# An attention and expert kernel on one core: code of k ahead of the products with v, additions and roundings of VectorE in two-input form, first heads in another order

## The chip, the cores and the metric

The kernel runs on one core of a Trainium2 chip. The metric is the device time of one execution in microseconds (us), the median of the runs shown. Five engines work side by side, each through its own queue in order, and wait for one another by semaphores: TensorE (PE; PEld are its weight loads), VectorE (DVE), ScalarE (ACT), GpSimd (POOL) and SyncE (SP, which only issues transfers here).

## What is computed

Attention over 16 heads (2 batches of 8), 768 rows of 64 each, in which a row of q sees only those rows of k whose six sign bits under a random projection are the same; then a layer of 8 experts with one expert per token; then a dense layer with ELU. The change touches the attention alone.

```python
q_bits = (np.einsum('bhsd,dk->bhsk', q, proj) > 0)      # 6 bits a row; k_bits likewise
mask = q_bucket[:, :, :, None] == k_bucket[:, :, None, :]
scores = np.where(mask, scale * q @ k.T, -1e9)
scores = scores - scores.max(-1)
attn = np.exp(scores); attn = attn / (attn.sum(-1) + 1e-09)
x = attn @ v          # then the experts, then moe2
```

## The kernel before

**Tiling.** A head has six score tiles of 128 rows (J = 6, HALF = 384 columns are one bank). Tile m is computed by `scores(m)` into pair_s or pair_t (L1202, eight matmul records, as fp32r high and low parts q_a, q_b, k_a, k_b), VectorE takes its negated maximum (`row_max`, L850), ScalarE the exponential with its row sum (`exp_rows`, L643), TensorE turns it (`turn_exps`, L1213, six transposes in two halves of three), ScalarE copies the first half out (`copy_t0`, L652) and VectorE the second (`copy_t1`, L873), and TensorE multiplies by v (`times_v`, L1228, 12 matmuls for half a head) and by the last weights (`last`, L1250).

**Preparing a head.** `project(g)` (L1172) makes the bits, `sign(g)` (L857, VectorE) makes them 0 or 1, `code(g, 0)` for q and `code(g, 1)` for k (L1184, TensorE) turn them into a code in bank_a (k's code of heads 0 and 1: bank_b). The code is read out by `mask_odd` on ScalarE (L628 for q, L630 for k) and `mask_even` on VectorE (L865). `high(g, c)` on VectorE (L843, L841) rounds q (c = 0) and k (c = 1) to fp32r; GpSimd copies and subtracts the roundings (`place_q`: L504, L506; `place_k`: L513, L515), scales k (L528), works on finished rows (`rows_of`, L487 to L495) and subtracts weight chunks (`w_lo`, L476).

**Denominators.** `inverse(u)` (VectorE) adds 1e-9 to the row sums den (L879, 128x6 values) and takes the reciprocal (L880).

**Order.** After a start written out by hand, a loop over n = 6 to 53 has three parts per head g = n // 3, each with two score tiles of head g - 1. The same loop stands on every engine, so that each queue's order is fixed. In part 1 of head g TensorE had: scores twice, `turn_exps(m_e)`, `times_v`, `turn_exps(m_e + 1)`, `code(g, 1)`. VectorE had in part 1: `copy_t1`, `mask_even(g, 0)`, `row_max` twice, `copy_t1`, `high(g + 1, 1)`, `mask_even(g, 1)`, `inverse(g - 2)`, and in part 2 first `copy_t1`, then `row_max`. `code(g, 1)` waits for both readers of `code(g, 0)`, since both codes lie in bank_a. `turn_exps(m)` waits for the first half before its first transpose, and for `copy_t1(m - 1)` before its fourth.

**Start.** `WARM_UP` is the number of matmuls on zeros (L1270) ahead of `project(0)` and ahead of `scores(0)`. `scores(0)` waits for all masks of head 0 and for the parts of q and k.

Of the kernel before, what the change touches and what calls it, by code (L numbers as in the profile page):

```python
# [22 lines left out]
ALU = mybir.AluOpType  # L23
# [10 lines left out]
EPS = 1e-9  # L34
# [5 lines left out]
HEADS = B * H  # L40
# [27 lines left out]
GROUPS = 3 * (HEADS + 2)  # L68
GROUP_S, GROUP_E = 3, 4
COPIES = 4  # L70
WARM_UP = (7, 10)
BIT_K = 32
BT = 3
NB = BT * P
# [56 lines left out]
def program(nc, q, k, v, proj, w_gate, w_ogate, w1, w2, w_in, w_out, const, out):  # L131
    with ExitStack() as ctx:
# [31 lines left out]
        with ExitStack() as att:  # L164
# [10 lines left out]
            raw = sb("raw", [P, 2, S])  # L175
# [94 lines left out]
        def turned_tile(m, part):  # L270
            a = (m // JH % 4) * HALF + m % JH * P
            return exps_t[:, part, a:a + P]
# [14 lines left out]
        s_hi, s_qa, s_ka = sem("s_hi"), sem("s_qa"), sem("s_ka")  # L287
# [185 lines left out]
        def _(pool):  # L473
# [41 lines left out]
                pool.tensor_tensor(k_b[top, g % 3, :], raw[low, g % 2, :], k_b[low, g % 3, :].bitcast(F32),  # L515
                                   ALU.subtract).then_inc(s_cp, 1)

            pool.wait_ge(s_hi, 1)
            pool.tensor_tensor(q_b[low, 0, :], raw[top, 0, :], q_b[top, 0, :].bitcast(F32), ALU.subtract).then_inc(s_cp, 1)
            pool.wait_ge(s_cp, prepared(0))  # L520
            for g in range(1, HEADS):
# [290 lines left out]
        def _(dve):  # L812
            chain = [0]

            def then(ins):

                chain[0] += 1
                ins.then_inc(s_dd, 1)
                dve.wait_ge(s_dd, chain[0])
# [11 lines left out]
            def high(g, c):  # L831
                at = (slice(0, D), slice(D, P))[c]
                if c == 0 or g == 0:
                    dve.wait_ge(s_raw[g % 2][c], 16 * (g // 2 + 1))
                else:
                    dve.wait_ge(s_ks, g)
                if g >= 3:
                    dve.wait_ge(s_sc, J * (g - 2))
                to = (q_b, k_b)[c][at, g % 3, :]
                if c == 1 and g == 0:  # L840
                    dve.tensor_scalar(to, raw[at, 0, :], SCALE, None, ALU.mult).then_inc(s_hi, 1)  # L841
                else:
                    dve.tensor_copy(to, raw[at, g % 2, :]).then_inc(s_hi, 1)  # L843

            def row_max(m):
                g, qt = place_of(m)
                dve.wait_ge(s_sc, m + 1)
                if g >= 2 and m % J == 0:
                    dve.wait_ge(s_ex, J * (g - 1))
                dve.tensor_reduce(nmax[:, g % 2, qt:qt + 1], score_pair[m % 2][:, :, 0:HALF], AX.XY, ALU.max,  # L850
                                  negate=True).then_inc(s_mx, 1)

            def sign(g):
                dve.wait_ge(s_bits, g + 1)
                if g >= 1:
                    dve.wait_ge(s_code, 2 * g)
                dve.tensor_scalar(bits[:, 0:QUART], bank_a[:, 0:QUART], 0.0, None, ALU.is_gt).then_inc(s_sgn, 1)  # L857

            def mask_even(g, c):
                dve.wait_ge(s_code, 2 * g + c + 1)  # L860
                if g == 0:
                    dve.wait_ge(s_id, 16)
                to = (q_a, k_a)[c][D:P, g % 3, :].rearrange("p (h o n) -> p o h n", h=2, o=2)[:, 0]
                coded = code_bank(g, c)[0:D, 0:HALF].rearrange("p (h n) -> p h n", h=2)
                dve.tensor_scalar(to, coded, popcount[0:D, :], BIG if c else -1.0,  # L865
                                  ALU.is_equal, ALU.mult if c else ALU.add).then_inc(s_mq, 1)

            def copy_t1(m):
                hh = m // JH
                if hh >= 4:  # L870
                    dve.wait_ge(s_av, (hh - 1) // 2)
                dve.wait_ge(s_pt, 2 * m + 2)
                dve.tensor_copy(turned_tile(m, slice(JH, J)),  # L873
                                exps_pair(m)[:, 1, 0:HALF].rearrange("p (j n) -> p j n", j=JH)).then_inc(s_t1, 1)

            def inverse(u):
                dve.wait_ge(s_ex, min(J * u + JH, J * HEADS))
                d = den[:, u % 4, parts_of(u)]
                then(dve.tensor_scalar(d, d, EPS, None, ALU.add))  # L879
                dve.reciprocal(d, d).then_inc(s_inv, 1)  # L880

            high(0, 0)
            high(0, 1)
            dve.wait_ge(s_hi, 2)
            dve.scalar_tensor_tensor(k_b[0:D, 0, :], raw[D:P, 0, :], SCALE, k_b[D:P, 0, :].bitcast(F32),
                                     ALU.mult, ALU.subtract).then_inc(s_lo, 1)
            sign(0)
            mask_even(0, 0)
            mask_even(0, 1)
            high(1, 0)  # L890
            high(1, 1)
            row_max(0)
            row_max(1)
            high(2, 0)

            row_max(2)
            copy_t1(0)
            row_max(3)
            high(2, 1)
            sign(1)  # L900

            copy_t1(1)
            row_max(4)
# [1 line left out]
            mask_even(1, 1)  # L905
            row_max(5)
            copy_t1(2)

            for n in range(6, GROUPS):
                g, part = n // 3, n % 3  # L910
# [247 lines left out]
        def _(pe):  # L1158
# [17 lines left out]
            def code(g, c):  # L1176
                pe.wait_ge(s_sgn, g + 1)
                if g == 0:
                    pe.wait_ge(s_setup, 2)
                if g >= 2 and c == 1:  # L1180
                    pe.wait_ge(s_mq, 2 * g + 1)
                    pe.wait_ge(s_mk, 2 * g + 1)
                for h in range(2):
                    mm = pe.matmul(code_bank(g, c)[:, h * QUART:(h + 1) * QUART], pat_bf[:, h, c, :], bits[:, 0:QUART],  # L1184
                                   start=True, stop=True)
                mm.then_inc(s_code, 1)

            def scores(m):
                g, qt = place_of(m)
                pe.wait_ge(s_mq, 2 * g + 2)  # L1190
                pe.wait_ge(s_mk, 2 * g + 2)
                pe.wait_ge(s_cp, prepared(g))
                if g == 0:
                    pe.wait_ge(s_lo, 1)
                    pe.wait_ge(s_qa, 1)
                    pe.wait_ge(s_ka, 1)
                if m >= 2:
                    pe.wait_ge(s_ex, m - 1)
                t = slice(qt * P, (qt + 1) * P)
                for a, b, first in ((q_a, k_a, True), (q_b, k_b, False)):  # L1200
                    for h in range(2):
                        mm = pe.matmul(score_pair[m % 2][:, h, 0:HALF], a[:, g % 3, t],  # L1202
                                       b[:, g % 3, h * HALF:(h + 1) * HALF], start=first, stop=not first)
                mm.then_inc(s_sc, 1)

            def turn_exps(m):
                pe.wait_ge(s_ex, m + 1)
                for part, free in enumerate((s_t0, s_t1)):
                    if 1 <= m < J * HEADS - 2:
                        pe.wait_ge(free, m)  # L1210
                    for n in range(JH):
                        kt = part * JH + n
                        mm = pe.transpose(exps_pair(m)[:, part, n * P:(n + 1) * P], exps[:, m % 4, kt * P:(kt + 1) * P],  # L1213
                                          ident)
                    mm.then_inc(s_pt, 1)
# [52 lines left out]
            def warm_up(stage):  # L1268
                for i in range(WARM_UP[stage]):
                    pe.matmul(pair_s[:, i % 2, 0:HALF], bits[:, 0:P], bits[:, :], start=True, stop=True)  # L1270
# [24 lines left out]
            for n in range(6, GROUPS):  # L1295
                g, part = n // 3, n % 3
                m_s, m_e = 2 * (n - GROUP_S), 2 * (n - GROUP_E)
                if m_s < J * HEADS:
                    scores(m_s)
                    scores(m_s + 1)  # L1300
                if n == 3 * HEADS + 3:
                    times_v(g - 2, 0)
                if 0 <= m_e < J * HEADS:
                    turn_exps(m_e)
                if n == 3 * HEADS + 3:
                    turn_exps(m_e + 1)
                if g == 2 and part == 1:
                    times_v_alone(0, 0, 0)
                if g >= 3 and part <= 1 and n != 3 * HEADS + 3:
                    times_v(g - 2, part)  # L1310
                if n == 3 * HEADS + 4:
                    times_v_alone(HEADS, HEADS - 1, 2 * HEADS - 1)
                if g == 2 and part == 2:
                    last_alone(0)
                if g >= 3 and part == 2:
                    last(g - 2)
                if n == 3 * HEADS + 5:
                    last_alone(HEADS)
                if 0 <= m_e < J * HEADS and n != 3 * HEADS + 3:
                    turn_exps(m_e + 1)  # L1320
                if g < HEADS and part < 2:
                    code(g, part)
                if g + 1 < HEADS and part == 2:
                    project(g + 1)

# [194 lines left out]
```

## Time and profile before

| quantity | value |
|---|---|
| median of 3 runs | 800.43 us (800.31 to 800.81) |
| the profiled execution | 800.52 us |
| its span in the trace | 798.7 us |
| TensorE busy | 766.0 us (96%) |
| VectorE busy | 452.0 us (57%) |
| ScalarE busy | 353.8 us (44%) |
| GpSimd busy | 368.8 us (46%) |

The span is shorter than the profiled execution by 1.8 us that lie around it. Attention ends at some 272 us of the span. Matmuls are pipelined and their ends are modelled, so that in a row of matmuls the next starts some 0.1 to 0.2 us before the end that is given for the last; starts are the better measure. Idle time in brackets is that of the engine just before a row, with what ended it.

### The profile page before, as it was taken

What the parts mean: (1) busy time and instruction counts of PE and PEld (TensorE: products, weight loads), DVE (VectorE), ACT (ScalarE), POOL (GpSimd) and SP (SyncE); (2) the same over time, 40 slices, a digit from 0 to 9 for tenths busy, and PEclk for the clock granted to TensorE, in tenths of its full rate; (3) what the DMA queues carried; (4) which work ended last, traced back from release to release, by engine and by line L of the source; (5) the groups of instructions that cost most, each with busy time, mean ns of one, the idle gap of its engine ahead of it and who ended that gap; (6) DMA issues with size and microseconds to landing.
All of it is one profiled execution on the core that took longest, in us unless ns stands there. A gap on an engine that the chain in (4) does not pass through costs nothing.

```text
span 798.7 us, 12417 instructions
## 1 busy us (share of the span) xinstructions
PE 766.0 (96%) x4269; PEld 630.2 (79%) x4269; DVE 452.0 (57%) x783; ACT 353.8 (44%) x661; POOL 368.8 (46%) x254
## 2 busy tenths in 40 slices
PE   6899989999999989999999999999999999999997
PEld 4666666666667678888888888899889889989985
DVE  7887777777776674544445445559427415613720
ACT  5766667766777421344323440057217305603610
POOL 5645564667761179977779883125310020000000
PEclk9999999999999999999999999999999999999999
DMA  5322233211110176775657750430010020000000
GB/s 141 110 82 67 79 91 83 54 40 50 41 40 11 26 269 233 251 234 161 202 177 229 233 176 27 153 138 1 27 53 1 1 67 14 0 14 27 1 14 26
DMA packets 39754, 72.79 MB, mean 91 GB/s; under 512 B 18768, under 2 KB 21072, under 8 KB 39696
## 3 DMA queue, kind: packets, MB, share of 16 engines
q1 hardware_dynamic: 26800, 29.19, 12.1%
q10 hardware_dynamic: 9456, 31.53, 12.1%
q0 software_dynamic: 3440, 11.28, 4.4%
q8 instruction: 38, 0.62, 0.3%
q14 instruction: 20, 0.16, 0.1%
HBM read 60.70 MB, written 11.28 MB: 90 GB/s over the span
## 4 chain that ended last, share of the span: by engine, by line
PE 54%; issue 28%; DVE 12%; POOL 2%; ACT 1%; DMA 1%; POOLq 0%; SPq 0%; DVEq 0%
PE pair_s L1389 13%; PE pair_t L1404 13%; PE bank_b L1228 7%; PE pair_u L1213 6%; DVE nmax L850 4%; PE pair_s L1202 3%; PE pair_t L1202 3%; PE pair_u L1368 2%; DVE exps_t L873 2%; DVE den L879 2%; DVE k_a L865 1%; POOL out L601 1%; PE pair_s L1441 1%; DVE g_lo L1148 1%; PE bank_a L1172 1%
## 5 line engine op out<-in xcount | busy, mean ns | idle before, releaser
L476 POOL TENSOR_TENSOR w_part<-w_raw,w_part 128x1024 fp32r<-128x1024 f32 x80 | 190.2, 2405 | 56.6 <-ACT w_part L702 56.4
L702 ACT ACTIVATE w_part<-w_raw 128x1024 fp32r<-128x1024 f32 x72 | 73.9, 1054 | 134.2 <-PE pair_t L1404 100.4
L1491 PE MATMUL pair_t<-w_part,g_hi 128*128 128x512 f32 x384 | 119.0, 391 | 0.3 <-POOL w_part L476 0.3
L1389 PE MATMUL pair_s<-w_part,xs_t 128*128 x456 | 108.7, 394 | 0.4 <-DVE xs_t L1026 0.4
L1404 PE MATMUL pair_t<-w_part,hid_t 128*128 x456 | 109.0, 394 | 0.0
L601 POOL DMA_INDIRECT out<-o_sb,token x12 | 11.7, 975 | 208.6 <-DVE o_sb L1118 208.6
L1213 PE MATMUL pair_u<-first,exps 128*128 128x128 f32 x564 | 85.6, 279 | 15.9 <-DVE exps_t L873 12.0
L1213 PEld LDWEIGHTS pair_u<-first,exps 128*128 128x128 f32 x564 | 63.0, 140 | 46.5 <-DVE exps_t L873 19.3
L1389 PEld LDWEIGHTS pair_s<-w_part,xs_t 128*128 128x128 f32 x456 | 84.2, 188 | 17.7 <-issue 0.9
L1404 PEld LDWEIGHTS pair_t<-w_part,hid_t 128*128 128x128 f32 x456 | 84.4, 188 | 16.9
L798 ACT ACTIVATE elu<-elu 128x384 f32<-128x384 f32 x64 | 33.6, 525 | 122.6 <-DVE elu L1138 122.5
L1491 PEld LDWEIGHTS pair_t<-w_part,g_hi 128*128 128x128 f32 x384 | 71.6, 188 | 15.1 <-issue 0.7
L1491 PE MATMUL pair_t<-w_part,g_lo 128*128 128x512 f32 x192 | 74.9, 390 | 0.0
L1441 PE MATMUL pair_u<-y_t,w_part 128*128 128x384 f32 x384 | 69.3, 334 | 0.3 <-DVE elu L1143 0.3
L652 ACT ACTIVATE exps_t<-pair_u 128x384 f32<-128x384 f32 x94 | 46.0, 490 | 52.7 <-PE pair_u L1213 52.7
L873 DVE COPY exps_t<-pair_u 128x384 f32<-128x384 f32 x94 | 51.5, 548 | 31.6 <-PE pair_u L1213 31.6
L1441 PE MATMUL pair_s<-y_t,w_part 128*128 128x384 f32 x384 | 69.3, 335 | 0.0
L1441 PEld LDWEIGHTS pair_u<-y_t,w_part 128*128 128x128 f32 x384 | 66.8, 188 | 0.7 <-DVE elu L1143 0.6
L1441 PEld LDWEIGHTS pair_s<-y_t,w_part 128*128 128x128 f32 x384 | 66.9, 188 | 0.2
L1044 DVE CAST hid_t<-pair_u 128x512 fp32r<-128x512 f32 x38 | 26.0, 685 | 67.2 <-PE pair_u L1368 67.2
L1228 PE MATMUL bank_b<-exps_t,v_nat 128*64 128x384 f32 x336 | 60.4, 494 | 0.0
L850 DVE TENSOR_REDUCE nmax<-pair_s 128x1 f32<-128x768 f32 x48 | 45.8, 954 | 12.7 <-PE pair_s L1202 12.0
(207 smaller groups left out, 1173.9 us busy)
## 6 DMA issues: line engine op xcount, KB each, us to landing
w_raw<-in_moe_w ACTq DMA_DIRECT2D x48, 512.0 KB, 6.5
w_raw<-in_moe_w SPq DMA_DIRECT2D x16, 512.0 KB, 8.5
ys_sorted<-ys SPq DMA_DIRECT2D x19, 256.5 KB, 3.6
w_raw<-in_moe_w_in ACTq DMA_DIRECT2D x8, 512.0 KB, 7.6
raw<-in_q SPq DMA_DIRECT2D x16, 192.0 KB, 3.2
raw<-in_k SPq DMA_DIRECT2D x16, 192.0 KB, 3.4
v_nat<-in_v SPq DMA_DIRECT2D x16, 192.0 KB, 2.4
x_rows<-rows_sb SPq DMA_DIRECT2D x32, 96.0 KB, 2.4
```

What stands on the lines that cost most here:

```text
L476: pool.tensor_tensor(chunk_of(w_part, n, 1, c), w_raw[n % 2][c][:, :], chunk_of(w_part, n, 0, c).bitcast(F32), ALU.subtract).then_inc(s_wl ...
L652: act.activation(turned_tile(m, slice(0, JH)), exps_pair(m)[:, 0, 0:HALF].rearrange("p (j n) -> p j n", j=JH), ACT.Copy).then_inc(s_t0, 1)
L702: act.activation(chunk_of(w_part, n, 0, c), w_raw[n % 2][c][:, :], ACT.Copy).then_inc(s_whi, 1)
L850: dve.tensor_reduce(nmax[:, g % 2, qt:qt + 1], score_pair[m % 2][:, :, 0:HALF], AX.XY, ALU.max, negate=True).then_inc(s_mx, 1)
L873: dve.tensor_copy(turned_tile(m, slice(JH, J)), exps_pair(m)[:, 1, 0:HALF].rearrange("p (j n) -> p j n", j=JH)).then_inc(s_t1, 1)
L1202: mm = pe.matmul(score_pair[m % 2][:, h, 0:HALF], a[:, g % 3, t], b[:, g % 3, h * HALF:(h + 1) * HALF], start=first, stop=not first)
L1213: mm = pe.transpose(exps_pair(m)[:, part, n * P:(n + 1) * P], exps[:, m % 4, kt * P:(kt + 1) * P], ident)
L1228: mm = pe.matmul(u_bank(u)[o * D:(o + 1) * D, 0:HALF], v_nat[:, (u - 1 + o) % 4, j, :], turned_half(2 * u - 1 + o)[:, j], start=j == 0, st ...
L1389: mm = pe.matmul(pair_s[:, h, :], xs_t[:, xp, c * P:(c + 1) * P], w_part[:, bass.ds(par, 1), wp, a:a + 512], start=c == 0 and xp == 0 and ...
L1404: mm = pe.matmul(pair_t[:, s % 2, :], hid_t[:, hp, c * P:(c + 1) * P], w_part[:, bass.ds(par, 1), wp, a:a + DM], start=c == 0 and n == 0, ...
L1441: mm = pe.matmul(hidden_bank[n % 4][:, 0:NB], w_in_p[:, wp, c, f * P:(f + 1) * P], y_t[:, yp, c, :], start=c == 0 and m == 0, stop=c == CD ...
L1491: mm = pe.matmul(pair_t[:, t % 2, :], gp[:, f, j * P:(j + 1) * P], w_out_p[:, wp, f, :], start=f == 0 and m == 0, stop=f == FT - 1 and m == 2)
```

## The change

Four things change. TensorE's `code(g, 1)` moves in part 1 of every head from behind the second `turn_exps` to ahead of `times_v`. VectorE's addition to den, and its roundings of heads 1 and 2, become scalar_tensor_tensor operations whose two tensor inputs are the same tensor. In the start, VectorE's roundings of heads 1 and 2 move, ten warm-up matmuls ahead of `scores(0)` become three, and GpSimd's first subtraction waits for the rounding of k of head 0 as well as for that of q.

```diff
-WARM_UP = (7, 10)
+WARM_UP = (7, 3)
...
-            pool.wait_ge(s_hi, 1)
+            pool.wait_ge(s_hi, 2)
...
                 to = (q_b, k_b)[c][at, g % 3, :]
-                if c == 1 and g == 0:
+                if 1 <= g <= 2:
+                    dve.scalar_tensor_tensor(to, raw[at, g % 2, :], 1.0, raw[at, g % 2, :], ALU.mult,
+                                             ALU.max).then_inc(s_hi, 1)
+                elif c == 1 and g == 0:
...
                 d = den[:, u % 4, parts_of(u)]
-                then(dve.tensor_scalar(d, d, EPS, None, ALU.add))
+                then(dve.scalar_tensor_tensor(d, d, EPS, d, ALU.add, ALU.max))
...
+                if g < HEADS and part == 1:
+                    code(g, 1)
                 if g == 2 and part == 1:
                     times_v_alone(0, 0, 0)
...
-                if g < HEADS and part < 2:
-                    code(g, part)
+                if g < HEADS and part == 0:
+                    code(g, 0)
```

TensorE, part 1 of head 3 (every later head is alike). L1202 are scores, L1213 transposes, L1228 the products with v, L1184 the code. Before:

```order
L1202 MATMUL pair_t<-k_b,q_b 128x384 x2
L1213 MATMUL pair_u<-first,exps 128x128 x6
L1228 MATMUL bank_b<-exps_t,v_nat 64x384 x6
L1213 MATMUL pair_u<-first,exps 128x128 x6
L1184 MATMUL bank_a<-bits,pat_bf 128x192 x2
L1202 MATMUL pair_s<-k_a,q_a 128x384 x2
```

TensorE, the same place after the change (the same lines are L1205, L1216, L1231 and L1187 there):

```order
L1205 MATMUL pair_t<-k_b,q_b 128x384 x2
L1216 MATMUL pair_u<-first,exps 128x128 x6
L1187 MATMUL bank_a<-bits,pat_bf 128x192 x2
L1231 MATMUL bank_b<-exps_t,v_nat 64x384 x6
L1216 MATMUL pair_u<-first,exps 128x128 x6
L1205 MATMUL pair_s<-k_a,q_a 128x384 x2
```

The two matmuls of k's code now stand before the products with v and one group of transposes, and nothing else of TensorE's loop moved.

VectorE at the start, from its first rounding on. Before:

```order
L843 CAST q_b<-raw 64x768
L841 TENSOR_SCALAR k_b<-raw 64x768
L885 SCALAR_TENSOR_TENSOR k_b<-raw,k_b 64x768
L857 TENSOR_SCALAR bits<-bank_a 128x192
L865 TENSOR_SCALAR q_a<-bank_a,first 64x2x192
L865 TENSOR_SCALAR k_a<-bank_b,first 64x2x192
L843 CAST q_b<-raw 64x768
L843 CAST k_b<-raw 64x768
L850 TENSOR_REDUCE nmax<-pair_s 128x1
L850 TENSOR_REDUCE nmax<-pair_t 128x1
L843 CAST q_b<-raw 64x768
L850 TENSOR_REDUCE nmax<-pair_s 128x1
```

VectorE, the same place after the change (L841 is now the two-input rounding, L853 the row maximum, L868 the mask):

```order
L846 CAST q_b<-raw 64x768
L844 TENSOR_SCALAR k_b<-raw 64x768
L888 SCALAR_TENSOR_TENSOR k_b<-raw,k_b 64x768
L860 TENSOR_SCALAR bits<-bank_a 128x192
L841 SCALAR_TENSOR_TENSOR q_b<-raw 64x768
L868 TENSOR_SCALAR q_a<-bank_a,first 64x2x192
L868 TENSOR_SCALAR k_a<-bank_b,first 64x2x192
L853 TENSOR_REDUCE nmax<-pair_s 128x1
L853 TENSOR_REDUCE nmax<-pair_t 128x1
L841 SCALAR_TENSOR_TENSOR k_b<-raw 64x768
L853 TENSOR_REDUCE nmax<-pair_s 128x1
```

The rounding of q of head 1 stands ahead of head 0's masks, that of k of head 1 behind the first two row maxima, and those of head 2 further back.

## Rows read from the trace of the kernel before

**Rows 1.** Groups by line and shape, span 0 to 300: count | busy us, mean ns | idle.

```profile
L873 DVE COPY exps_t<-pair_u 128x384 f32<-128x384 f32 x94 | 51.5, 548 | 31.6 <-PE pair_u L1213 31.6
...
L879 DVE TENSOR_SCALAR den<-den 128x6 f32<-128x6 f32 x15 | 14.1, 938 | 0.4
...
L865 DVE TENSOR_SCALAR k_a<-bank_a,first 64x384 fp32r<-64x384 f32 x14 | 8.5, 610 | 16.5 <-PE bank_a L1184 16.5
```

**Rows 2.** Timeline, TensorE over one head: start us, duration us, work [idle before].

```profile
147.29 0.60 PE L1202 MATMUL pair_s<-k_a,q_a 128*128 128x384 f32 x2
...
149.16 0.52 PE L1213 MATMUL pair_u<-first,exps 128*128 128x128 f32 x3 [0.23 <-ACT exps_t L652]
...
150.05 0.55 PE L1213 MATMUL pair_u<-first,exps 128*128 128x128 f32 x3 [0.37 <-DVE exps_t L873]
...
150.43 0.98 PE L1250 MATMUL bank_b<-last_w,u_sb 128*128 128x160 f32 x6
...
151.25 0.49 PE L1213 MATMUL pair_u<-first,exps 128*128 128x128 f32 x3
...
152.24 0.55 PE L1213 MATMUL pair_u<-first,exps 128*128 128x128 f32 x3 [0.50 <-DVE exps_t L873]
...
153.18 0.62 PE L1202 MATMUL pair_s<-k_a,q_a 128*128 128x384 f32 x2
...
158.33 0.60 PE L1202 MATMUL pair_s<-k_a,q_a 128*128 128x384 f32 x2
...
159.81 0.82 PE L1213 MATMUL pair_u<-first,exps 128*128 128x128 f32 x6
...
160.56 2.16 PE L1228 MATMUL bank_b<-exps_t,v_nat 128*64 128x384 f32 x12
```

**Rows 3.** The same timeline, VectorE and GpSimd around k's code and the denominators.

```profile
154.18 0.96 DVE L850 TENSOR_REDUCE nmax<-pair_s 128x1 f32<-128x768 f32 x1 [0.73 <-PE pair_s L1202]
...
159.08 0.61 DVE L865 TENSOR_SCALAR q_a<-bank_a,first 64x384 fp32r<-64x384 f32 x1
...
162.04 0.56 DVE L843 CAST k_b<-raw 64x768 fp32r<-64x768 f32 x1
...
162.73 0.82 POOL L513 CAST k_a<-k_b 64x768 fp32r<-64x768 f32 x1 [2.67 <-DVE k_b L843]
...
163.64 1.84 POOL L515 TENSOR_TENSOR k_b<-raw,k_b 64x768 fp32r<-64x768 f32 x1
...
163.72 0.61 DVE L865 TENSOR_SCALAR k_a<-bank_a,first 64x384 fp32r<-64x384 f32 x1 [1.12 <-PE bank_a L1184]
...
164.36 1.14 DVE L879 TENSOR_SCALAR den<-den 128x6 f32<-128x6 f32 x1
```

**Rows 4.** Timeline, VectorE and GpSimd where GpSimd's copy meets a cast.

```profile
44.08 0.82 POOL L504 CAST q_a<-q_b 64x768 fp32r<-64x768 f32 x1 [5.82 <-DVE q_b L843]
44.15 0.83 DVE L931 CAST iota_bf<-cst 128x128 bf16<-128x128 f32 x1
```

**Rows 5.** Timeline, last layer, where w_lo meets a subtraction with two SBUF inputs.

```profile
538.98 2.39 POOL L476 TENSOR_TENSOR w_part<-w_raw,w_part 128x1024 fp32r<-128x1024 f32 x1 [1.44 <-ACT w_part L702]
539.01 2.79 DVE L1148 TENSOR_TENSOR g_lo<-elu,g_hi 128x384 fp32r<-128x384 f32 x1
```

**Rows 6.** Timeline, the start.

```profile
4.82 2.08 DVE L841 TENSOR_SCALAR k_b<-raw 64x768 fp32r<-64x768 f32 x1 [0.24 <-DMA raw<-in_k]
...
6.93 0.95 DVE L885 SCALAR_TENSOR_TENSOR k_b<-raw,k_b 64x768 fp32r<-64x768 f32 x1
...
8.82 3.41 PE L1270 MATMUL pair_s<-bits 128*128 128x384 bf16 x10
...
9.29 0.60 DVE L865 TENSOR_SCALAR k_a<-bank_b,first 64x384 fp32r<-64x384 f32 x1
...
11.78 1.09 PE L1202 MATMUL pair_s<-k_a,q_a 128*128 128x384 f32 x2
...
13.45 0.96 DVE L850 TENSOR_REDUCE nmax<-pair_s 128x1 f32<-128x768 f32 x1 [2.27 <-PE pair_s L1202]
```

More of the change, by code:

```diff
@@ L887, in _ @@
             sign(0)
+            high(1, 0)
             mask_even(0, 0)
             mask_even(0, 1)
-            high(1, 0)
-            high(1, 1)
             row_max(0)
             row_max(1)
-            high(2, 0)
+            high(1, 1)
             row_max(2)
@@ L898, in _ @@
             row_max(3)
-            high(2, 1)
             sign(1)
+            high(2, 0)
             copy_t1(1)
@@ L907, in _ @@
             copy_t1(2)
+            high(2, 1)
             for n in range(6, GROUPS):
```

## The prediction, made before the changed kernel was run

> **What bounds the kernel now.** I read the groups by line first, then one head of the timeline, then the start. After attention the change touches nothing, so I leave those 526 us as they are. Within attention TensorE is dense but for one place per head. The groups show what is odd on VectorE: the addition of a constant to 128x6 numbers takes 938 ns on average, 15 times, and the mask of k's code makes VectorE sit idle for 16.5 us in 14 heads, waiting for TensorE's code [rows 1]. The timeline shows what both cost. In the 5.89 us from the scores at 147.29 to the next part's scores at 153.18, TensorE waits three times, for 0.23, 0.37 and 0.50 us, each time for a copy of the transposes by ScalarE or VectorE [rows 2]. The other two parts of a head have no such wait: scores at 158.33, transposes at 159.81, products at 160.56 [rows 2].
>
> The waits come from a queue. VectorE ends its rounding of k at 162.60 and then stands until 163.72 for the code; mask, addition and reciprocal follow, and only then the copy and the row maxima that TensorE and ScalarE need [rows 3]. The addition starts at 164.36 and takes 1.14 us, to 165.50, while GpSimd's L515 runs from 163.64 to 165.48 [rows 3]: it ends with GpSimd's work. VectorE cannot run this operation while GpSimd holds something that both need.
>
> **Part 1: the two-input form.** Does it free VectorE from GpSimd? The trace has a two-input operation that reads both inputs from SBUF: L1148 starts at 539.01, 0.03 us behind GpSimd's L476, and ends at 541.80, 0.43 us behind L476's end at 541.37 [rows 5]. So it too waited for GpSimd and then did its work. I take the form alone at 0 us for the denominators. Were it free of GpSimd, the 15 additions would fall from 0.94 us [rows 1] to what is left, at least zero, and the form alone would return up to 14 us; nothing in the rows supports that.
>
> On this the Trainium skill has a rule ("SBUF — State Buffer", section on the two separate sides): VectorE and GpSimd share a port pair as an exclusive lock, and a VectorE operation with two SBUF inputs takes it against a GpSimd operation that reads SBUF, as one in a 2-port mode does. By that rule the title's first edit gains nothing at the denominators, without it up to 14 us; the trace agrees with the rule (2.79 us at 539.01 [rows 5]).
>
> The early roundings cost more in the new form if nothing blocks: the same shape in two-input form is 0.95 us [rows 6], the cast 0.56 [rows 3]. Three of the four lie behind other work or ahead of waits; I take 0 to +0.8 us in all and keep it in the start's bounds.
>
> **Part 2: the code ahead of the products.** The two matmuls are the same, so TensorE's own work stays. The code is then ready ahead of the 2.16 us of products [rows 2], so VectorE's mask starts when the rounding ends, at 162.60 in place of 163.72, and ends at 163.21. The addition asks at 163.24. GpSimd's L513 runs then, to 163.55, and L515 follows only at 163.64 [rows 3]. Does the addition get in between? A case of just this kind is there: the cast L931 asked at 44.15 under GpSimd's copy L504 (44.08 to 44.90) and was done at 44.98 [rows 4], 0.08 us after that copy's end, in a gap like that between L513 and L515. So the addition ends at some 163.6 in place of 165.50. With some 0.2 for the reciprocal and 0.55 for the copy [rows 1], VectorE is free at about 164.4. The scores are ready for the row maximum 1.00 us after their start (153.18 to 154.18 [rows 2, 3]); the scores of this head's part 2 start about 0.1 behind the last code of the timeline, at 163.5, one 16.18 us period behind 147.29. So they are ready at 164.5, and VectorE is no longer late.
>
> What is late next? TensorE itself, without waits: scores to transposes 1.48 us (158.33 to 159.81), six transposes 0.75 (to 160.56), `last` 0.82 (150.43 to 151.25), three transposes 0.37 (half of 0.75), the rest with the projection 0.94 (152.24 to 153.18) [rows 2]. That is 4.36 us where now 5.89 pass: 1.53 us per head. The nearest other bound is VectorE's copy that the last three transposes need: row maxima at 164.5, two of 0.96, one copy of 0.55 [rows 1, 3], overlapped by some 0.15, so 166.8 to 166.95; TensorE arrives at 163.5 + 1.48 + 0.75 + 0.82 + 0.37 = 166.9. That is even, so I take 1.45 of the 1.53. The lower bound for this term is the sum of the three waits as the rows give it, 1.10 us per head; less if a new wait appears.
>
> What hides the rest: GpSimd starts its share of k with the rounding, which does not move against TensorE; its idle 2.67 us before L513 [rows 3] covers the shorter period. ScalarE's mask of k gains in the same way, which takes away the first of the three waits. SP's transfers are released by the projection a head ahead. Heads 3 to 14 are regular: 12 x 1.45 = 17.4 us. In head 2 GpSimd is behind, because the rounding of k of head 2 now comes last of the start; the addition there can meet a subtraction of 1.84 us [rows 3] for most of its length. I give head 2 only 0.5 us of the 1.5. Head 15 I leave at zero.
>
> The added wait: `code(g, 1)` waits for the masks of q's code before the products. VectorE's mask ends at 159.08 + 0.61 = 159.69, and TensorE arrives at 160.56 [rows 2, 3]. Behind it would be queued the products, transposes and the next scores. Cover is 0.87 us, cost nothing.
>
> **Part 3: the start.** The ten warm-up matmuls take 3.41 us from 8.82 and end where `scores(0)` starts, at 11.78; the last mask of VectorE was done at 9.29 + 0.60 = 9.89 [rows 6]. With three, TensorE is ready at some 9.8 and the masks decide. Rounding k at 4.82 took 2.08 us since GpSimd ran [rows 6]; now GpSimd waits for it, so it takes 0.56 and ends at 5.4. L885 adds 0.95 (6.4), the sign some 0.35 (6.75), then the new rounding of head 1: 0.95 if free (7.7), or, if GpSimd's subtraction of 1.84 us begun at 6.4 holds it, to 8.2 + 0.8 = 9.0. Two masks of 0.61 give 8.9 to 10.2. By part 1 I take 10.2. `scores(0)` then starts 1.6 us earlier, and the first row maximum at 11.85 in place of 13.45. Behind that, VectorE no longer stands blocked in a rounding between row maxima; I take 0.2 for it. The start: -1.8 us, with bounds -2.9 (no lock) and +1.0 (next paragraph but one, the clock).
>
> **Sum.** 800.5 (profiled execution, equal to the median of 800.43 within 0.1) - 1.8 - 0.5 - 17.4 = 780.8 us.
>
> **Rivals.**
> (B) Part of the waits remain. The balance with VectorE's copy is even to 0.1 us, and ScalarE's copies follow close behind. If a head returns only 0.8 to 1.1 us (the modelled waits and less), 13 heads give 10 to 14 us, with the start 785 to 789; I take 787. For: three engines are nearly balanced. Against: no row shows another late engine.
> (C) The addition loses the gap to L515. It would then end at 165.5 as before and all that follows on VectorE stays where it was; only the start is gained: 798.7. Against it stands L931 [rows 4].
> (D) The form does what its words suggest and runs beside GpSimd. Then the addition ends 0.35 us earlier, but the scores are not ready before 164.5, so steady heads gain nothing more; the start gains 1 us: 779.8. The reason differs, the time lies inside my forecast's range.
> (E) Slower: the new wait of `code(g, 1)`. It costs once q's mask on VectorE is over 0.87 us later than now against TensorE, and makes a head slower than before once it is over 0.87 + 1.45 = 2.3 us late. VectorE's rounding of q stands ahead of it and can be held by GpSimd's w_lo and the scaling of k behind it; at 2.39 us each [rows 5] that is up to 4.8 us. In the six heads with a w_lo this would cost (4.8 - 2.3) x 6 = 15 us; with the start, head 2 and the other six heads' 8.7 us returned, 800.5 + 15 - 11.0 = 804.5. Against: GpSimd stands idle for 2.67 us before each rounding of k releases it [rows 3], so it is not behind its work by that much.
> (The clock.) The warm-up matmuls are 0.34 us apart, against 0.18 for scores of the same 384 columns later [rows 2, 6], so TensorE runs at the lower of its two levels (1.2 and 2.4 GHz) until about 12.5 us, after work without a pause from 8.2, although the granted clock column reads 1.00. With less of that work it may rise later. A set of scores costs some 0.65 us more at the lower level; with four of them on the path, +2.6 against the start's -1.8. This widens the range up by 1 to 2 us and is not a case of its own.
>
> **How the numbers follow.** Forecast (with D) 0.72, its own range 777.5 to 784; B 0.14; C 0.07; E 0.04; the rest, unnamed, 0.03. The range 777.5 to 788.5 holds the forecast and most of B, some 0.8. What a measurement here can tell from no change is about 0.2%, 1.6 us, so 798.8 is the edge: C lies on it and is split. Faster 0.89, same 0.07, slower 0.04.
>
> **What would show it.** Right: VectorE's idle before the mask of k gone (16.5 us before), the addition to den at 0.3 to 0.4 us from its start, not 0.94; scores of a part 0 following those of part 2 by 4.4 us, not 5.89; period of a head 14.7 us, not 16.18; the first row maximum near 11.9. Wrong: additions that still end with L515 (C); additions of 0.15 us with L513 running beside (D); TensorE waiting in front of L1187 (E); TensorE waits of over 0.2 us for exps_t in most heads (B).

## The result and the profile after

The changed kernel takes 778.39 us (median of 4 runs, 776.54 to 779.32) against 800.62 us of the kernel before in the same runs: ratio 0.972, 95% interval 0.9698 to 0.9741. I had forecast 780.8 us. The profiled execution took 779.32 us, with a span of 777.5 us (798.7 before). The experts' first layer starts at 265.50 us in place of 286.72: all of the 21.2 us lies ahead of it, in the attention.

The groups of the kernel after, span 0 to 300 (count | busy us, mean ns | idle before), answer to [rows 1]; L876, L868 and L882 are L873, L865 and L879 of before:

```profile
L876 DVE COPY exps_t<-pair_u 128x384 f32<-128x384 f32 x94 | 51.9, 552 | 29.9 <-PE pair_u L1216 29.8
...
L868 DVE TENSOR_SCALAR k_a<-bank_a,first 64x384 fp32r<-64x384 f32 x14 | 8.5, 610 | 0.5
...
L882 DVE SCALAR_TENSOR_TENSOR den<-den 128x6 f32<-128x6 f32 x15 | 4.1, 276 | 0.4
```

The mask of k's code no longer waits (0.5 us idle in place of 16.5), and the addition takes 276 ns on average, not 938. One head's timeline of the kernel after shows how (start, duration, work, idle before); it answers to [rows 2, 3]:

```profile
106.03 0.56 DVE L846 CAST k_b<-raw 64x768 fp32r<-64x768 f32 x1
...
106.62 0.61 DVE L868 TENSOR_SCALAR k_a<-bank_a,first 64x384 fp32r<-64x384 f32 x1
...
106.72 0.82 POOL L513 CAST k_a<-k_b 64x768 fp32r<-64x768 f32 x1 [2.67 <-DVE k_b L846]
...
107.26 0.30 DVE L882 SCALAR_TENSOR_TENSOR den<-den 128x6 f32<-128x6 f32 x1
...
107.42 0.60 PE L1205 MATMUL pair_s<-k_a,q_a 128*128 128x384 f32 x2
...
107.62 1.84 POOL L515 TENSOR_TENSOR k_b<-raw,k_b 64x768 fp32r<-64x768 f32 x1
107.77 0.56 DVE L876 COPY exps_t<-pair_u 128x384 f32<-128x384 f32 x1
...
108.90 0.82 PE L1216 MATMUL pair_u<-first,exps 128*128 128x128 f32 x6
...
109.56 0.98 PE L1253 MATMUL bank_b<-last_w,u_sb 128*128 128x160 f32 x6
...
110.37 0.92 PE L1216 MATMUL pair_u<-first,exps 128*128 128x128 f32 x6
...
111.69 0.62 PE L1205 MATMUL pair_s<-k_a,q_a 128*128 128x384 f32 x2
```

The addition asks at 107.26 under GpSimd's copy L513 (to 107.54), ends at 107.56 and so gets in before L515 starts at 107.62. VectorE operations that read what TensorE has written, in PSUM, do not wait here: the mask at 106.62 takes 0.61 us under L513, as with GpSimd idle (0.60 at 9.29 [rows 6]), and the copy at 107.77 takes 0.56 us under L515. The addition reads SBUF, as GpSimd's operations do. TensorE goes from the scores at 107.42 to those at 111.69 in 4.27 us, with no wait, where 5.89 us passed before [rows 2]. The next part 2 starts at 121.95, so a head takes 14.53 us in place of 16.18.

### The profile page after: what moved, and what is told of

Its sections match the earlier page's. It is cut to its first block, busy times and chain, and to the rows that moved or that the text cites. A ratio compares the mean times of both kernels' runs of the same rounds, so it can differ in the third digit from the quotient of the medians.

```text
span 777.5 us, 12403 instructions
## 1 busy us (share of the span) xinstructions
PE 759.5 (98%) x4262; PEld 632.0 (81%) x4262; DVE 447.3 (58%) x783; ACT 354.0 (46%) x661; POOL 369.5 (48%) x254
## 4 chain that ended last, share of the span: by engine, by line
PE 60%; issue 29%; DVE 5%; POOL 2%; ACT 1%; DMA 1%; SPq 0%; POOLq 0%; DVEq 0%
PE pair_s L1394 13%; PE pair_t L1409 13%; PE pair_u L1216 8%; PE bank_b L1231 8%; PE pair_s L1205 5%; PE pair_t L1205 4%; PE pair_u L1373 2%; PE bank_b L1253 1%; POOL out L601 1%; DVE nmax L853 1%; PE pair_s L1446 1%; DVE g_lo L1151 1%; PE bank_a L1175 1%; POOL y_raw L595 1%; DVE exps_t L876 1%
## 5 line engine op out<-in xcount | busy, mean ns | idle before, releaser
L476 POOL TENSOR_TENSOR w_part<-w_raw,w_part 128x1024 fp32r<-128x1024 f32 x80 | 190.3, 2405 | 56.7 <-ACT w_part L702 56.5
L1216 PEld LDWEIGHTS pair_u<-first,exps 128*128 128x128 f32 x564 | 64.9, 141 | 24.8 <-ACT exps L643 17.2
L1216 PE MATMUL pair_u<-first,exps 128*128 128x128 f32 x564 | 81.7, 279 | 2.1 <-DVE exps_t L876 1.6
L652 ACT ACTIVATE exps_t<-pair_u 128x384 f32<-128x384 f32 x94 | 46.1, 490 | 54.4 <-PE pair_u L1216 54.4
L876 DVE COPY exps_t<-pair_u 128x384 f32<-128x384 f32 x94 | 51.9, 552 | 29.9 <-PE pair_u L1216 29.8
L1231 PE MATMUL bank_b<-exps_t,v_nat 128*64 128x384 f32 x336 | 60.4, 494 | 0.0
L853 DVE TENSOR_REDUCE nmax<-pair_s 128x1 f32<-128x768 f32 x48 | 45.9, 957 | 13.6 <-PE pair_s L1205 12.1
```

Source lines behind the costliest of these rows:

```text
L476: pool.tensor_tensor(chunk_of(w_part, n, 1, c), w_raw[n % 2][c][:, :], chunk_of(w_part, n, 0, c).bitcast(F32), ALU.subtract).then_inc(s_wl ...
L652: act.activation(turned_tile(m, slice(0, JH)), exps_pair(m)[:, 0, 0:HALF].rearrange("p (j n) -> p j n", j=JH), ACT.Copy).then_inc(s_t0, 1)
L876: dve.tensor_copy(turned_tile(m, slice(JH, J)), exps_pair(m)[:, 1, 0:HALF].rearrange("p (j n) -> p j n", j=JH)).then_inc(s_t1, 1)
L1231: mm = pe.matmul(u_bank(u)[o * D:(o + 1) * D, 0:HALF], v_nat[:, (u - 1 + o) % 4, j, :], turned_half(2 * u - 1 + o)[:, j], start=j == 0, st ...
```

## The experiments

Each kernel is given with its edit, what was expected of it, and what came out. "Tile 6" is the start of the first scores of the loop, at 25.16 us in the trace of before and 24.91 after.

### The code's place alone

The kernel before, with `code(g, 1)` moved and nothing else.

```diff
+                if g < HEADS and part == 1:
+                    code(g, 1)
                 if g == 2 and part == 1:
                     times_v_alone(0, 0, 0)
...
-                if g < HEADS and part < 2:
-                    code(g, part)
+                if g < HEADS and part == 0:
+                    code(g, 0)
```

> The kernel before with one edit: TensorE's code of k ahead of the products with v; additions, roundings and start as before. Theory (the queue order is all of it): the addition to den meets only GpSimd's copy, 0.3 us in its old form too, a head takes 14.53 us instead of 16.18, and the whole gain of the steady heads is there: 779 to 781 us. Rival (the two-input form frees VectorE from GpSimd and carries a good part): additions stay near 1 us, 788 us or more.

777.47 us (777.07 to 778.89), ratio 0.972 (0.9701 to 0.9738): the whole gain. Its group of additions, in the old one-input form:

```profile
L879 DVE TENSOR_SCALAR den<-den 128x6 f32<-128x6 f32 x15 | 4.2, 282 | 0.4
```

282 ns, against 276 in the two-input form after. A head takes 14.53 us here too. One edit of the four makes the result; the other three add nothing that the intervals can show.

### The two-input addition alone

```diff
-                then(dve.tensor_scalar(d, d, EPS, None, ALU.add))
+                then(dve.scalar_tensor_tensor(d, d, EPS, d, ALU.add, ALU.max))
```

> The kernel before with one edit: the addition to den as a two-input operation. Theory (two inputs in SBUF wait for GpSimd as well): additions stay at 1.1 us in heads 2 to 14, time 800.6, no change. Rival (the form frees VectorE): additions of 0.2 us, a head shorter by 0.9 to 1.1 us, 787 to 789 us.

799.31 us (798.63 to 800.91) against 799.51 of before in the same runs; ratio 0.9998 (0.9987 to 1.0008). The group, and one head's timeline beside GpSimd:

```profile
L879 DVE SCALAR_TENSOR_TENSOR den<-den 128x6 f32<-128x6 f32 x15 | 14.0, 933 | 0.4
```

```profile
163.62 1.84 POOL L515 TENSOR_TENSOR k_b<-raw,k_b 64x768 fp32r<-64x768 f32 x1
...
164.35 1.15 DVE L879 SCALAR_TENSOR_TENSOR den<-den 128x6 f32<-128x6 f32 x1
```

The addition with two inputs still ends with L515 (165.50 and 165.46). The form does not free VectorE from GpSimd.

### The old addition in the kernel after

```diff
-                then(dve.scalar_tensor_tensor(d, d, EPS, d, ALU.add, ALU.max))
+                then(dve.tensor_scalar(d, d, EPS, None, ALU.add))
```

> The kernel after with the addition to den in its old one-input form. Theory: no difference, 777 to 779.5 us, additions of 0.31 us. Rival (the form is worth something once the code is early): 1 us or more slower than the kernel after.

779.06 us (778.92 to 779.95), ratio 0.974 (0.9724 to 0.9756), an interval that overlaps the one of the kernel after (0.9698 to 0.9741). The additions take 281 ns on average and a head 14.53 us in both. Neither place shows a worth of the form.

### The addition moved away from L515, the code left late

The kernel before, with the addition and the reciprocal of `inverse` moved to part 2 and nothing else.

```diff
                 if 0 <= m_e < J * HEADS:
                     copy_t1(m_e)
+                if part == 2 and g >= 2:
+                    inverse(g - 2)
...
-                if part == 1 and g >= 2:
-                    inverse(g - 2)
```

> The kernel before with one edit: addition and reciprocal of the denominators moved on VectorE from the end of part 1 to behind the row maxima of part 2; the code of k stays late. It tells how much of the 1.65 us per head the blocked addition alone makes. Theory: VectorE's row maximum comes 1.1 us earlier, TensorE's two waits for VectorE's copies go, that for ScalarE's copy (0.23 us by the trace, 0.4 by starts) stays: a head takes 15.0 to 15.2 us, 785 to 788 us. Rival (the wait for the code is the whole loss, the addition only fills it): at least 796 us.

782.92 us (782.25 to 784.34), ratio 0.9796 (0.9776 to 0.9815). Faster than either theory had it: a head takes 14.94 us (parts 0 start at 66.83 and 81.77). So of the 1.65 us per head the blocked addition made 1.24, and the late code, by way of ScalarE's mask, the remaining 0.41. The groups show it: the idle for the code is all there, the addition is short, and what TensorE still waits for is ScalarE's copy.

```profile
L1213 PE MATMUL pair_u<-first,exps 128*128 128x128 f32 x564 | 80.5, 278 | 4.5 <-ACT exps_t L652 3.6 <-DVE exps_t L873 0.8
...
L865 DVE TENSOR_SCALAR k_a<-bank_a,first 64x384 fp32r<-64x384 f32 x14 | 8.5, 611 | 16.5 <-PE bank_a L1184 16.5
...
L879 DVE TENSOR_SCALAR den<-den 128x6 f32<-128x6 f32 x15 | 2.7, 182 | 0.0
```

The timeline shows the way: ScalarE's mask L630 comes late, its copy L652 stands behind it (123.21 to 123.69), and the transposes wait for that copy.

```profile
122.22 0.58 ACT L630 ACTIVATE k_a<-bank_a,first 64x384 fp32r<-64x384 f32 x1 [1.07 <-PE bank_a L1184]
...
123.84 0.84 PE L1213 MATMUL pair_u<-first,exps 128*128 128x128 f32 x6 [0.23 <-ACT exps_t L652]
```

The 0.41 us can be had only once the addition is free: the kernel of the next section has the code early and the addition blocked, and a head takes 16.18 us again. Its second mask does not matter for that, since the addition ends with L515 either way, 2.07 us behind the scores there (83.44) and 2.03 us behind them before (165.50).

The misjudged part of the expectation was how much the start-to-start loss at VectorE's copies exceeds the idle that the rows give (0.37 + 0.50 = 0.87 us, measured 1.24).

### How near the edge the gain stands

The kernel after, with the mask of k's code written twice, so that the addition asks 0.6 us later.

```diff
+                if c == 1 and g >= 2:
+                    then(dve.tensor_scalar(to, coded, popcount[0:D, :], BIG,
+                                           ALU.is_equal, ALU.mult))
                 dve.tensor_scalar(to, coded, popcount[0:D, :], BIG if c else -1.0,
                                   ALU.is_equal, ALU.mult if c else ALU.add).then_inc(s_mq, 1)
```

> The kernel after with VectorE's mask of k's code written twice from head 2 on, which lets the addition to den ask some 0.6 us later, when GpSimd's subtraction L515 is under way. Theory (what frees the addition is only that it asks before L515 starts, 0.4 us ahead of it): the addition ends with L515 again, 1.1 to 1.6 us long, in two-input form as it is; a head takes 16.1 to 16.4 us and the kernel 797 to 801 us, all of the gain gone for 0.6 us of work per head. Rival (the two-input form or the early code frees VectorE for good): 14 x 0.6 us lie beside TensorE's work or cost at most 8 us, 778 to 786 us.

798.49 us (797.81 to 799.21), ratio 0.9984 (0.9971 to 0.9997). Its timeline:

```profile
80.57 0.61 DVE L869 TENSOR_SCALAR k_a<-bank_a,first 64x384 fp32r<-64x384 f32 x1
80.67 0.82 POOL L513 CAST k_a<-k_b 64x768 fp32r<-64x768 f32 x1 [2.67 <-DVE k_b L846]
...
81.21 0.61 DVE L871 TENSOR_SCALAR k_a<-bank_a,first 64x384 fp32r<-64x384 f32 x1
81.37 0.60 PE L1208 MATMUL pair_s<-k_a,q_a 128*128 128x384 f32 x2
81.57 1.84 POOL L515 TENSOR_TENSOR k_b<-raw,k_b 64x768 fp32r<-64x768 f32 x1
...
81.86 1.58 DVE L885 SCALAR_TENSOR_TENSOR den<-den 128x6 f32<-128x6 f32 x1
...
87.29 0.62 PE L1208 MATMUL pair_s<-k_a,q_a 128*128 128x384 f32 x2
```

The second mask itself does not wait (0.61 us at 81.21). The addition asks at 81.86, 0.29 us behind the start of L515, and ends with it (83.44 and 83.41). From 81.37 to the next part's scores 5.92 us pass, as before the change. With all four edits in place, 0.6 us of work per head takes back 20 of 22 us.

Is it the place or the work? The same kernel, with `inverse` moved behind the row maxima as above:

> The kernel with the doubled mask, and addition and reciprocal moved behind the row maxima of part 2, away from GpSimd's L515. Theory (the doubled mask cost 20 us only by sending the addition into L515, its own 0.6 us lie beside TensorE's work): a head takes 14.5 to 14.7 us again, 777 to 781 us, with the same extra work as in the kernel at 798.5. Rival (VectorE's queue has no room for the second mask): 786 us or more.

778.08 us (777.53 to 778.67), ratio 0.9726 (0.9709 to 0.9743), with the second mask still in it. The head from 91.09 to 105.64 takes 14.55 us. The work was all but free; the collision cost 20 us. In one head the second mask does cost something: from 105.64 it is 4.59 us to the next part's scores, 0.33 more than in the others. The same head is 0.34 us longer than the others with the doubled mask alone (16.52 us from 103.48), so this does not come from moving `inverse`. The moved addition does still meet GpSimd's row work L495 in 11 heads and takes 0.55 us there, but nothing waits for it.

### The start alone

The kernel after without its edits to the loop and to the addition.

```diff
-WARM_UP = (7, 10)
+WARM_UP = (7, 3)
...
-            pool.wait_ge(s_hi, 1)
+            pool.wait_ge(s_hi, 2)
...
-                if c == 1 and g == 0:
+                if 1 <= g <= 2:
+                    dve.scalar_tensor_tensor(to, raw[at, g % 2, :], 1.0, raw[at, g % 2, :], ALU.mult,
+                                             ALU.max).then_inc(s_hi, 1)
+                elif c == 1 and g == 0:
...
```

with the order of VectorE's start as in the change.

> The kernel after without its edits to the loop: only the start is new (three warm-up matmuls, roundings reordered and in two-input form, GpSimd's later wait). Theory (TensorE starts 1.4 us earlier but stays at its lower clock some 6 us longer): 799.5 to 800.8 us, varying from run to run more than before. Rival (the start is worth what I forecast): 798.8 us. In the trace scores of tile 6 start near 24.9 us as in the profile after, against 25.16 before.

799.06 us (796.72 to 799.38), ratio 0.9986 (0.9974 to 0.9997): 0.2 to 2.1 us faster, 1.1 by the middle, between the two expectations. In its trace tile 6 starts at 24.64, 0.5 us earlier than before, and head 2, which follows, is another 0.6 us shorter. Starts in us, one execution each:

| kernel | tile 6 (head 2, part 0) | head 3, part 0 | head 2 takes |
|---|---|---|---|
| before | 25.16 | 39.92 | 14.76 |
| the code's place alone | 25.35 | 38.62 | 13.27 |
| the start alone | 24.64 | 38.80 | 14.16 |
| after | 24.91 | 39.05 | 14.14 |

The two gains do not add up: alone, the start brings head 3 forward by 1.12 us and the code's place by 1.30, both together by 0.87.

Where the start's 1.6 us go is seen in the kernel after, by starts on TensorE and the roundings:

```profile
5.10 0.56 DVE L844 TENSOR_SCALAR k_b<-raw 64x768 fp32r<-64x768 f32 x1 [0.61 <-DMA raw<-in_k]
...
5.69 0.95 DVE L888 SCALAR_TENSOR_TENSOR k_b<-raw,k_b 64x768 fp32r<-64x768 f32 x1
5.74 2.58 POOL L519 TENSOR_TENSOR q_b<-raw,q_b 64x768 fp32r<-64x768 f32 x1 [5.30 <-DVE k_b L844]
...
6.95 2.19 DVE L841 SCALAR_TENSOR_TENSOR q_b<-raw 64x768 fp32r<-64x768 f32 x1
...
10.36 1.01 PE L1205 MATMUL pair_s<-k_a,q_a 128*128 128x384 f32 x2 [1.61 <-DVE k_a L868]
...
14.17 0.98 PE L1205 MATMUL pair_s<-k_a,q_a 128*128 128x384 f32 x2 [0.89 <-ACT exps L643]
...
16.72 0.99 PE L1205 MATMUL pair_t<-k_a,q_a 128*128 128x384 f32 x2
...
19.43 0.60 PE L1205 MATMUL pair_s<-k_a,q_a 128*128 128x384 f32 x2
```

The two-input rounding L841 asks at 6.95 under L519, which ends at 8.32, and ends at 9.14, 0.82 us later: it too waited. The scores start at 10.36, 1.4 us earlier than before [rows 6], but a pair of score matmuls takes 1.0 us at 10.36, 14.17 and still at 16.72, and 0.60 from 19.43 on. Before, the pace had risen with the scores of tile 1, at 13.25.

### Warm-up matmuls

Two kernels change the warm-up of the kernel after: `WARM_UP = (7, 10)`, and `WARM_UP = (12, 10)`, which leaves TensorE no pause between the first warm-up and the projection (the pauses behind it, of 1.06 and 1.25 us, stay).

> The kernel after with ten warm-up matmuls ahead of the first scores, as before. Theory (TensorE's clock rises after a stretch of work, and three matmuls leave it low until about 19 us): scores(0) start at 10.9, 0.5 us later than after, but the clock is up from about 12.5 us as in the kernel before; 776.5 to 778 us, 0 to 1.5 us faster than after and steadier. Rival (the clock costs nothing on the path): 0.5 us slower than after.

777.22 us (775.55 to 777.50), ratio 0.9709 (0.9691 to 0.9726); tile 6 at 22.87, 2.0 us earlier than in the kernel after. The first scores start at 10.41, hardly later than the 10.36 after three matmuls, and their second pair takes 0.56 us.

> The kernel after with twelve and ten warm-up matmuls in place of seven and three: TensorE works without a long pause from 1.1 us on. Theory: the clock rises before scores(0), which then start at 10.4 and take 1.0 us to the first row maximum in place of 1.65, and the whole start runs at the upper clock: 775.5 to 777 us. Rival (the clock costs nothing on the path): as the kernel after, 778.

776.37 us (775.18 to 776.96), ratio 0.9702 (0.9685 to 0.9718); tile 6 at 22.00, 2.9 us earlier. Its start:

```profile
1.12 3.85 PE L1273 MATMUL pair_s<-bits 128*128 128x384 bf16 x12 [1.12 <-DVE bits L821]
5.05 0.53 PE L1175 MATMUL bank_a<-raw,proj_w 128*32 128x192 f32 x8
...
6.98 1.79 PE L1273 MATMUL pair_s<-bits 128*128 128x384 bf16 x10
10.02 0.62 PE L1205 MATMUL pair_s<-k_a,q_a 128*128 128x384 f32 x2 [1.25 <-DVE k_a L868]
```

The projection takes 0.53 us, not the 0.87 of the kernel after, and ten warm-up matmuls 1.79 us, not 3.41: TensorE is at its upper level from 5 us on. In the times the step from three to ten matmuls is 1.2 us and the intervals of the ratios overlap, so the times alone do not tell it from nothing.

A trace shown above in part tells more. The kernel with the doubled mask and `inverse` moved has the start of the kernel after, line for line, with three warm-up matmuls; its edits begin behind tile 6. In its execution the pace had risen by 14.46:

```profile
10.65 1.01 PE L1208 MATMUL pair_s<-k_a,q_a 128*128 128x384 f32 x2 [1.60 <-DVE k_a L871]
...
14.46 0.59 PE L1208 MATMUL pair_s<-k_a,q_a 128*128 128x384 f32 x2 [0.89 <-ACT exps L643]
...
23.54 0.59 PE L1208 MATMUL pair_s<-k_a,q_a 128*128 128x384 f32 x2
```

Its first scores start 0.3 us later than in the kernel after, and still its tile 6 starts 1.4 us earlier. The lead arises where the pace has doubled: from the scores of tile 2 to the projection behind them 2.22 us pass (14.46 to 16.68), in the kernel after 4.11 us (14.17 to 18.28). So the rival that the clock costs nothing falls. It also shows that three matmuls do not always leave the clock low that long: four of the five executions traced with this start had it low until about 18 us, this one only until about 14.

The same long warm-up on the kernel before with the code moved, that is with the old roundings in their old order:

```diff
-WARM_UP = (7, 10)
+WARM_UP = (12, 10)
```

> The kernel before with the code of k ahead, and twelve and ten warm-up matmuls; roundings as before. Against e9 it tells what reordered early roundings are worth with the clock up in both. Theory: scores(0) start near 10 to 11.8 us; the roundings of head 1 stand in front of the first row maxima and the one at 15.3 us blocks on GpSimd, so 0.5 to 1.5 us slower than e9: 776.5 to 778 us.

777.52 us (775.52 to 778.41), ratio 0.9712 (0.9693 to 0.9731). In its trace the clock had not risen before the scores: twelve matmuls take 4.02 us, but the projection 0.87 and ten matmuls 3.41 us, with scores at 11.76 and tile 6 at 25.38. So the run does not compare the roundings at the same clock. It shows instead that behind the same twelve matmuls the clock was up in one execution and not in another.

At last the long warm-up with the reordered early roundings in their old form:

```diff
-                if 1 <= g <= 2:
-                    dve.scalar_tensor_tensor(to, raw[at, g % 2, :], 1.0, raw[at, g % 2, :], ALU.mult,
-                                             ALU.max).then_inc(s_hi, 1)
-                elif c == 1 and g == 0:
+                if c == 1 and g == 0:
```

> The kernel with twelve and ten warm-up matmuls, with the early roundings of heads 1 and 2 in their old one-input form at their new places. Theory (both forms wait for GpSimd, the old one works at twice the pace): the rounding of q of head 1 ends 0.4 us earlier, scores(0) start at 9.6 to 9.7 in place of 10.0, tile 6 at 21.0 to 22.0 in place of 22.0; 775.5 to 776.5 us, the same or up to 1 us faster than with the two-input form. Rival (the two-input form avoids a wait for GpSimd): slower by 0.5 to 1.5 us, with a cast of over 2 us at the start.

775.25 us (775.20 to 776.03), ratio 0.9689 (0.9676 to 0.9702): the lowest median of the study. Its own cast beside GpSimd:

```profile
5.49 2.57 POOL L519 TENSOR_TENSOR q_b<-raw,q_b 64x768 fp32r<-64x768 f32 x1 [5.05 <-DVE k_b L841]
...
6.69 1.78 DVE L843 CAST q_b<-raw 64x768 fp32r<-64x768 f32 x1
```

The cast ends 0.41 us behind L519 (8.47 and 8.06), the two-input form 0.82 us behind it in the kernel after: both wait, and what the cast has left to do takes half as long. Tile 6 starts at 21.96 against 22.00, although this execution was at the lower level through the projection (0.87 us) and nearly all of the ten matmuls (3.34 us). Against the two-input form with the same warm-up (0.9702) the intervals overlap, so that I call it not slower, and no more.

## Why the prediction was right

**Part 1, the two-input form at nothing: right.** 799.31 against 799.51 us with that edit alone, additions of 933 ns in place of 938 [rows 1]. The row that carried it, L1148 behind L476 [rows 5], was the right one to read. Rival D falls by this and by the start's L841. (Where the prediction speaks of the title's first edit in this place, the additions in two-input form are meant.)

**Part 2, the queue: right in mechanism and nearly in size.** Forecast, with what was measured in brackets: addition done 0.3 to 0.4 us from its start (0.30), scores to scores 4.4 us (4.27), period 14.7 us (14.53). I gave 1.45 us per head for heads 3 to 14; it was 1.65, as the stretch from head 3's part 0 (39.92 before, 39.05 after) to head 15's (234.13 and 213.41) shortened by 19.85 us. Two terms were mis-sized. The time from six transposes to the next work I took at 0.75 us from a place with the products behind them; ahead of `last` it is 0.66 (108.90 to 109.56). And the 0.08 us that I held back for VectorE's copy was not needed: the copy at 110.14 ends at 110.69 and the transposes do not wait.

**Rival C did not happen, but stands close by.** The addition got into the gap, as the cast at 44.15 had [rows 4]; it asks 0.36 us ahead of L515. The doubled mask delayed it by 0.64 us, past that gap, and cost what C had named, all of the gain in heads 3 to 14. Where between the two the gain is lost was not measured.

**Heads 2 and 15.** Head 2 gave 0.62 us where I had 0.5, and the number is luck: I counted it for the early code, but the start alone makes head 2 0.60 us shorter, and the early code adds 0.02 to that. With the old start the early code gives 1.49 us (the table above). What takes them away is what I had named: GpSimd is behind, and the addition meets a subtraction, in the kernel after

```profile
33.17 2.02 POOL L506 TENSOR_TENSOR q_b<-raw,q_b 64x768 fp32r<-64x768 f32 x1
...
34.17 1.03 DVE L882 SCALAR_TENSOR_TENSOR den<-den 128x3 f32<-128x3 f32 x1
```

Head 15, which I left at zero, and what follows it gave 0.5 (from 20.7 at its part 0 to 21.2 at the experts), by the code's place: the kernel with the doubled mask has that head in 13.98 us as well (before 14.60), the one with only `inverse` moved in 14.43.

**The start: a term that failed in size.** I forecast -1.8 us. Up to the first row maximum that was nearly right (12.04 where I had 11.85, and 13.45 before). But in the profiled execution tile 6 moves by only 0.25 us; the runs with the start alone are some 1.1 us faster, of which their trace has 0.5 by tile 6. The step that failed is that I put the clock into the bounds only. With seven warm-up matmuls fewer, the pieces of TensorE work that followed ran at half pace in this execution: the scores of tiles 1 to 3 took some 0.65 us more each (for tile 2 1.42 us from its start to the next work at 14.17, 0.78 us at 15.58 before). The terms err against each other: 1.55 us too much at the start, 3.05 us too little in the heads (2.45 in heads 3 to 14, 0.1 in head 2, 0.5 from head 15), together the 1.5 us by which the profiled execution (779.32) lies below 780.8. The median of its runs is 0.9 us lower still. That the sum came so near is in part luck.

**Rivals B and E** have nothing for them: TensorE's idle for copies is 2.1 us over all transposes in the kernel after, where it was 0.23, 0.37 and 0.50 in each head [rows 2], and L1187 waits for no mask in the loop.

**What stays open.** What decides when TensorE's clock rises in the start was not settled: it varies between executions with the same code. The start's part of the gain is smaller than the spread of the runs. A collision of the kind that the loop had can be a part of it. The two kernels with only the addition changed or moved share the old start; their traces reach tile 6 at 23.27 (moved) and 25.19 (changed). With the addition moved, the cast of q asks 0.27 us ahead of GpSimd's L515 and gets in; in the other it asks 0.05 us behind its start and waits:

```profile
14.42 0.60 DVE L843 CAST q_b<-raw 64x768 fp32r<-64x768 f32 x1
...
14.69 2.03 POOL L515 TENSOR_TENSOR k_b<-raw,k_b 64x768 fp32r<-64x768 f32 x1
```

```profile
14.70 1.83 POOL L515 TENSOR_TENSOR k_b<-raw,k_b 64x768 fp32r<-64x768 f32 x1
...
14.75 2.20 DVE L843 CAST q_b<-raw 64x768 fp32r<-64x768 f32 x1
```

## What to carry to other kernels

A tiny operation, of 0.16 us where it runs alone (182 ns on average in the kernel that moves it), cost 1.24 us per head, not by its work but by where in the queue it stood: just behind the start of another engine's 1.8 us. Before changing such an operation's form, look at what ends it: if it ends with another engine's work, change when it asks, and measure how far it then stands from the next collision (here 0.36 us). One wait can also hide another: the wait for the code was worth 0.41 us per head, but only once the addition no longer waited. One edit here, moving two matmuls, took both away. To move the addition to part 2 as well would take the gain off that edge: the kernel with both moves takes 778.08 us with the second mask in it.

## What the runs showed of the hardware

- A VectorE operation with two inputs in SBUF waits for a running GpSimd operation just as one with one input does: 933 and 938 ns for the same 128x6 addition, 2.19 us for a rounding of 0.95 us. VectorE operations that read PSUM did not wait: 0.61 us for the mask and 0.56 us for the copy, with L513 or L515 running. The waiting goes both ways: GpSimd's L519, 1.81 us in the kernel before, took 2.58 us when L888 had started 0.05 us ahead of it.
- A waiting VectorE operation gets its turn in the 0.08 us between two dependent GpSimd operations (107.54 to 107.62), in each of heads 3 to 14 (0.30 or 0.31 us for every addition).
- TensorE's pace doubles some way into the start, and the moment varies with the same code. With three warm-up matmuls ahead of the scores a pair of scores still took 0.99 us at 16.72 us in one execution and 0.59 us at 14.46 in another. With twelve matmuls in place of seven at the very start the upper level was there at 5 us in one execution, between 10 and 11 us in a second, and only behind 12 us in a third. The profile's granted clock reads 1.00 all the while; only durations show it.
